# Products of a tile of ones on TensorE in the opening of a gated-attention and two-MLP kernel

## The reference, cut to what matters

```python
# attention, per batch (4) and head (8), 768 tokens, head size 48
for t in range(S):
    state = f[t][:, None] * state + outer(k[t], v[t])      # f = sigmoid(f_logit)
    y[t] = q[t] @ state
# first MLP on x (4, 768, 384): 384 -> 1536 -> 384, with a residual
xn = (x - mean) / sqrt(var + 1e-6) * g_ln
x = x + relu(xn @ w_ch1) @ w_ch2
# second MLP: 384 -> 1024 -> 384, with a gate from a convolution over 3 tokens
h = relu(x @ w_in)
out = (h * sigmoid(conv3(h, conv_w))) @ w_out
```

## Time and profile before

| | |
|---|---|
| median of 3 runs | 728.15 us (725.46 to 732.2) |
| the profiled execution | 729.54 us |
| its span, first to last instruction | 727.5 us |
| mean granted TensorE clock | 0.979 |
| TensorE busy in the span | 696.6 us (96%) |
| VectorE, ScalarE, GpSimd busy | 476.9, 311.6, 157.3 us |

### The profile page before, as it was taken

How to read it: one execution, slowest core, us unless ns; L and a number is a source line. 1 busy time by engine, 2 the same in 40 slices (tenths; PEclk the granted TensorE clock), 3 DMA queues, 4 the chain that set the end, 5 groups by cost and what they waited for, 6 DMA issues and landing times.

```text
span 727.5 us, 21762 instructions
## 1 busy us (share of the span) xinstructions
PE 696.6 (96%) x9616; PEld 651.1 (90%) x9616; DVE 476.9 (66%) x885; ACT 311.6 (43%) x604; POOL 157.3 (22%) x178
## 2 busy tenths in 40 slices
PE   4878899999999999999999999999999999999998
PEld 3556699999999999999999999999989999999997
DVE  2774886557765856765865863435387777777764
ACT  3262631341242251261151142224477676776764
POOL 4021503143333423423414414500000000000000
PEclk9769999999999999999999999999999999999999
DMA  8322520432152133332342112135010120220111
GB/s 330 128 99 97 180 90 3 186 121 100 59 196 108 59 128 116 120 121 90 106 170 88 57 57 88 57 103 179 33 38 31 45 75 1 75 75 1 37 39 38
DMA packets 23231, 67.71 MB, mean 93 GB/s; under 512 B 3809, under 2 KB 14817, under 8 KB 23137
## 3 DMA queue, kind: packets, MB, share of 16 engines
q1 hardware_dynamic: 23136, 66.32, 26.5%
HBM read 56.86 MB, written 9.45 MB: 91 GB/s over the span
## 4 chain that ended last, share of the span: by engine, by line
PE 90%; DVE 5%; issue 2%; DMA 2%; ACT 1%; SPq 0%; DVEq 0%; ACTq 0%
PE bank L1118 14%; PE bank L1120 13%; PE bank L1119 13%; PE bank L1313 9%; PE bank L1015 9%; PE bank L1315 9%; PE bank L1314 9%; PE bank L1037 4%; DMA F<-f 2%; PE bank L1089 2%; PE bank L1059 2%; PE bank L1031 1%; PE bank L951 1%; PE bank L1112 1%; PE bank L1100 1%
## 5 line engine op out<-in xcount | busy, mean ns | idle before, releaser
L705 ACT ACTIVATE HHI<-bank 128x384 fp32r<-128x384 f32 x96 | 47.2, 492 | 160.0 <-PE bank L1120 159.7
L1290 DVE SCALAR_TENSOR_TENSOR TB<-HB,CW,TB 128x440 f32<-128x440 f32 x112 | 75.8, 677 | 50.2 <-ACT TB L1253 48.2
L917 DVE SCALAR_TENSOR_TENSOR HLO<-bank,HHI 128x384 fp32r<-128x384 f32 x96 | 53.2, 554 | 83.7 <-ACT HHI L705 83.7
L1118 PE MATMUL bank<-HHI,W2H 128*128 128x384 f32 x288 | 100.6, 349 | 0.0
L1118 PE MATMUL bank<-XH,W1H 128*128 128x384 f32 x288 | 99.1, 344 | 0.0
L1120 PE MATMUL bank<-XH,W1L 128*128 128x384 f32 x288 | 96.5, 335 | 0.0
L1120 PE MATMUL bank<-HHI,W2L 128*128 128x384 f32 x288 | 96.5, 335 | 0.0
L1119 PE MATMUL bank<-XL,W1H 128*128 128x384 f32 x288 | 96.4, 335 | 0.0
L1119 PE MATMUL bank<-HLO,W2H 128*128 128x384 f32 x288 | 96.4, 335 | 0.0
L793 DVE TENSOR_TENSOR K<-K,TOT 128x768 f32<-128x768 f32 (+2 forms) x54 | 56.7, 1052 | 47.4 <-PE bank L1015 37.0
L1015 PEld LDWEIGHTS bank<-Q,K 48*64 48x64 f32 x3840 | 65.9, 144 | 22.0 <-issue 21.9
(11 more groups left out here) (127 smaller groups left out, 1373.5 us busy)
## 6 DMA issues: line engine op xcount, KB each, us to landing
NEAR<-near SPq DMA_DIRECT2D x21, 960.0 KB, 4.7
Q<-q SPq DMA_DIRECT2D x7, 768.0 KB, 4.3
K<-k SPq DMA_DIRECT2D x7, 768.0 KB, 4.9
F<-f SPq DMA_DIRECT2D x7, 768.0 KB, 6.1
V<-v SPq DMA_DIRECT2D x8, 576.0 KB, 6.9
x2d<-X SPq DMA_DIRECT2D x8, 576.0 KB, 4.4
XB<-x2d SPq DMA_DIRECT2D x6, 663.0 KB, 5.9
out<-OB SPq DMA_DIRECT2D x6, 660.0 KB, 4.4
```

The costliest lines, as they stand in the source:

```text
L705: nc.scalar.activation(HHI[:, g % RA], ub[g % 2][:, 0:T], ACT.Relu).then_inc(hh_ready, 1)
L917: nc.vector.scalar_tensor_tensor(out=HLO[:, g % RA], in0=ub[g % 2][:, 0:T], scalar=0.0, in1=HHI[:, g % RA].bitcast(F32), op0=ALU.max, op1= ...
L1118: mm(dst, ah, bh, start=start, stop=False, **kw)
L1290: nc.vector.scalar_tensor_tensor(out=TB[:, g % RB], in0=HB[:, g % RB, tap:tap + TB_], scalar=CW[:, g, tap:tap + 1], in1=TB[:, g % RB], op0 ...
```

## The change

`START` gets 36 `warm` steps, all of TensorE. Each consists of two products of 128x128 on 384 columns, but the first, in front of everything, of 20. Three steps stand behind each of `even0.a`, `even0.0` and `odd0.a`, two behind `odd0.0`, and two in front of each of the twelve `score` steps of unit 0 (`.a` and `.0`). All other steps keep their order. No wait is added but that of the first `warm` for `still_ready`. In all 90 products are added.

```diff
+        WARM_FIRST = 20
...
         START = placed("""
-            gates1.a gates1.0 even0.a whi0.0 diag0.0 even0.0 baseK0.a baseK0.0 baseQ0.a odd0.a baseQ0.0 pT0.a
-            odd0.0 whi1.0 pT0.0 self0.a wsub0.0 wlo0.0 wsub1.0 wlo1.0 score0.a wlo2.0 gates0.1 score0.0 pQ0.0
...
+            warm0.0 gates1.a gates1.0 even0.a warm1.0 warm2.0 warm3.0 whi0.0 diag0.0 even0.0 warm4.0 warm5.0
+            warm6.0 baseK0.a baseK0.0 baseQ0.a odd0.a warm7.0 warm8.0 warm9.0 baseQ0.0 pT0.a odd0.0 warm10.0
+            warm11.0 whi1.0 pT0.0 self0.a wsub0.0 wlo0.0 wsub1.0 wlo1.0 warm12.0 warm13.0 score0.a wlo2.0
+            gates0.1 warm14.0 warm15.0 score0.0 pQ0.0 wsub2.0 pQ0.a self0.0 pK1.a wsub3.0 gates1.1 warm16.0
+            warm17.0 score1.0 whi2.0 wsub4.0 warm18.0 warm19.0 score1.a whi3.0 pK1.0 warm20.0 warm21.0
+            score2.0 wlo3.0 copy3.0 pT1.a warm22.0 warm23.0 score2.a wsub5.0 whi4.0 warm24.0 warm25.0 score3.a
+            pT1.0 mask0.0 warm26.0 warm27.0 score3.0 mask0.a pQ1.0 pQ1.a baseK0.1 copy3.a near0.1 pK2.0 pT2.0
+            wlo4.0 mask1.0 pQ2.0 pK2.a pT2.a warm28.0 warm29.0 score4.0 mask1.a warm30.0 warm31.0 score4.a
+            pQ2.a pK3.0 pK3.a warm32.0 warm33.0 score5.0 mask2.a whi5.0 pT3.a pT3.0 warm34.0 warm35.0 score5.a
+            pQ3.a wsub6.0 ktr0.0 copy4.0 pQ3.0 wsub7.0 wlo5.0 mask2.0 pK4.a pK4.0 pT4.0 pT4.a pQ4.0 copy4.a
...
                 if i == 0:
                     pe.wait_ge(still_ready, 1)
-                for _ in range(2):
+                for _ in range(WARM_FIRST if i == 0 else 2):
                     mm(yb[:, 0:T], HLO[:, 0, 0:P], HLO[:, 0], start=True, stop=True)
```

More of the change, by code:

```diff
@@ L363, in phase_a @@
         START = placed("""
-            gates1.a gates1.0 even0.a whi0.0 diag0.0 even0.0 baseK0.a baseK0.0 baseQ0.a odd0.a baseQ0.0 pT0.a
-            odd0.0 whi1.0 pT0.0 self0.a wsub0.0 wlo0.0 wsub1.0 wlo1.0 score0.a wlo2.0 gates0.1 score0.0 pQ0.0
-            wsub2.0 pQ0.a self0.0 pK1.a wsub3.0 gates1.1 score1.0 whi2.0 wsub4.0 score1.a whi3.0 pK1.0
-            score2.0 wlo3.0 copy3.0 pT1.a score2.a wsub5.0 whi4.0 score3.a pT1.0 mask0.0 score3.0 mask0.a
-            pQ1.0 pQ1.a baseK0.1 copy3.a near0.1 pK2.0 pT2.0 wlo4.0 mask1.0 pQ2.0 pK2.a pT2.a score4.0 mask1.a
@@ L369, in phase_a @@
[L369 to L378, removed]
@@ L379, in phase_a @@
-            up2.0 pK5.1 up3.0 up4.0 neary1.1 baseK0.2 wlo13.0 ktr0.1 y0.1 pT5.1 xh1.0 gates1.2 copy3.1 pQ5.1
-            hlo0.0 baseQ0.2 kv0.1 pK6.1 xh2.0 pT6.1 pow0.1 hlo1.0 wlv9.0 hlo2.0 yend0.1 pQ6.1 sscale0.1
+            warm0.0 gates1.a gates1.0 even0.a warm1.0 warm2.0 warm3.0 whi0.0 diag0.0 even0.0 warm4.0 warm5.0
+            warm6.0 baseK0.a baseK0.0 baseQ0.a odd0.a warm7.0 warm8.0 warm9.0 baseQ0.0 pT0.a odd0.0 warm10.0
+            warm11.0 whi1.0 pT0.0 self0.a wsub0.0 wlo0.0 wsub1.0 wlo1.0 warm12.0 warm13.0 score0.a wlo2.0
@@ new lines, in phase_a @@
+            pQ2.a pK3.0 pK3.a warm32.0 warm33.0 score5.0 mask2.a whi5.0 pT3.a pT3.0 warm34.0 warm35.0 score5.a
+            pQ3.a wsub6.0 ktr0.0 copy4.0 pQ3.0 wsub7.0 wlo5.0 mask2.0 pK4.a pK4.0 pT4.0 pT4.a pQ4.0 copy4.a
+            wsub8.0 score0.1 baseQ0.1 y0.0 pK5.0 pQ4.a pT5.0 copy5.0 wlo6.0 kv0.0 pQ5.0 yend0.0 pK5.a wlo7.0
+            pT5.a pQ5.a pK6.0 ktok0.0 pK6.a pT6.0 pT6.a wlo8.0 neary0.1 copy5.a pQ6.a pQ6.0 wsub9.0 pT0.1
+            pQ0.1 nsum0.1 ktr1.0 wsub10.0 score1.1 pK1.1 wlo9.0 xadd0.0 ktok1.0 mask0.1 y1.0 pT1.1 kv1.0 pQ1.1
@@ new lines, in phase_a @@
+            yend1.0 wsub11.0 st0.0 xnt0.0 norm0.0 y2.0 wlo10.0 pow0.0 xadd1.0 pK2.1 sscale1.0 xn0.0 st1.0
+            mask1.1 pT2.1 sscale2.0 pQ2.1 xl0.0 gates0.2 yend2.0 xh0.0 score2.1 ktr2.0 whi6.0 wsub12.0 kv2.0
+            xadd2.0 wsub13.0 norm1.0 wsub14.0 xnt1.0 score3.1 wsub15.0 norm2.0 mask2.1 ktok2.0 xacc0.0 xnt2.0
+            pow1.0 xn1.0 pK3.1 st2.0 pT3.1 pQ3.1 pow2.0 near1.1 xacc1.0 xl1.0 xn2.0 score4.1 pK4.1 pT4.1
+            wlo11.0 up0.0 up1.0 pQ4.1 nsum1.1 xacc2.0 whi7.0 wlv8.0 score5.1 wlo12.0 azero0.2 whi8.0 xl2.0
@@ L381, in phase_a @@
+            down0.0 up2.0 pK5.1 up3.0 up4.0 neary1.1 baseK0.2 wlo13.0 ktr0.1 y0.1 pT5.1 xh1.0 gates1.2 copy3.1
+            pQ5.1 hlo0.0 baseQ0.2 kv0.1 pK6.1 xh2.0 pT6.1 pow0.1 hlo1.0 wlv9.0 hlo2.0 yend0.1 pQ6.1 sscale0.1
             wlo14.0 pT0.2 wlv10.0 hlo3.0 pQ0.2 down1.0 score0.2 wlo15.0 wlv11.0 down2.0 xadd0.1 whi9.0 st0.1
```

## The result

| | median | lowest to highest |
|---|---|---|
| changed kernel, 20 executions | 731.56 us | 729.16 to 736.18 |
| kernel before, 20 executions | 726.75 us | 724.16 to 732.20 |

The account below looks back on a forecast made before the run. TensorE, 90% of the chain, was taken to bound the kernel. Gains of 0.3, 2.5, 0.95 and 0.6 made 4.35 us, less 0.9 for holes, plus 0.5 at 57 us: 4.0 gained, median 724.1, range 718.5 to 735.5.

Parts of the forecast that it names:

- (c): From 25.8 to 38.65 us, TensorE alone: 12.85 us becomes 10.1, pairs 18 to 27 costing 3.4 of 6.1; gain 2.5.
- The 20 in front: Opening products, ending at 7.8 us under cover of the loads: cost nothing and raise the clock by 8 us.
- (a): From even0.0 at 10.68 us through odd0.0, which ends at 15.3 instead of 15.8: gain 0.3 us.
- (b): Up to 25.8 us, where VectorE sets the pace: pairs 10 to 17 are covered; without cover they would cost 2.7.
- The holes: Waits without a releaser in the short products, up to four of 0.45 us: 0 to 1.8 lost, 0.9 taken.
- the prediction's signs: List of what would show it right, among them fourth-level copies at 35.6 us and the dense part from about 82.7.
- (d): At score4.0: 1.97 us becomes 1.02, the pairs about it lying in waits for ScalarE and VectorE; gain 0.95.
- (f): Seventh weight split gains 1.1 us, but VectorE's Q for score0.1 is only 0.7 ahead: gain 0.6.
- (e): At score5: 48 short products fall by some 0.7 us and pair 34/35 costs 0.7: no gain.
- the low stretch at 57 us: Low clock from 57 to 60.2 us, no pair there: 0 to 1.6 us gained, 0.5 taken.
- The first: Rival: clock low for three tenths of (c) makes pairs lose; low at 10.68 us costs another 3.6; 738 us, chance 0.14.
- the ramp penalty: Low stretches across the opening, to 84.1 us: some 13 us by the rows, against 7.3 at most by the skill.

## Why the prediction was wrong

The place was right in the main: the end follows the start of the dense part (640.0 to 640.8 us long in the three profiles of this and of the kernel before, 639.9 to 643.4 in the experiments), and (c) got shorter. The sign was wrong. That the measured 731.56 lies between 718.5 and 735.5 is owed to the width of this range; the forecast within it was 724.1. Term by term:

**The 20 in front.** Costed at nothing; they end at 7.55, under the cover named, and the clock is high behind them, as forecast. Right by its mechanism. By themselves they bring no gain (1.0027).

**(a) and (b), gain 0.3 and nothing lost: a loss of 2.1 us at score1.0.** This is the first step that failed. Odd0.0 ends at 16.9 and not at 15.3. Six products take 1.31 us behind short ones and not 1.0, and the stream breaks for 0.69 us ahead of even0.0 and for 1.30 us inside odd0.0. Then the clock fell at 17, so that four products and a split run at half speed, and the chain stays on TensorE, holes included, until score0.0 ends at 24.4, where it had been VectorE's from 16 to 19.8: pairs 10 to 15, which (b) had covered, are on the path. The run without the token pairs starts score1.0 1.6 us earlier, but its time doesn't confirm the gain. With only score pairs, score1.0 starts at 26.5 instead of 26.1, so that (b) by itself was nearly right.

**The holes, 0 to 1.8 taken as 0.9.** Ahead of score0.1 the chain of the changed kernel has 3.2 us of them, against 0.9 in the earlier trace rows (0.48 and 0.45): 2.3 more, beyond the bound. I had them only in the score steps behind 28 us. The one in odd0.0 stands behind its 54th product in all four profiles with this order of instructions on 384 columns up to there (1.30, 0.76, 1.01 and 0.96 us: the changed kernel, and without 18 to 27, without 30 to 35, and without score pairs). The opening with 16 columns has the same order at the low clock and no hole there, and no other order or count has one in odd0.0. The falling of the clock at 17 is in two of these four.

**(c), gain 2.5: a gain of 1.6.** The mechanism and the sign are right, the size is off in two terms that partly cancel. The clock is worth 3.4 us there and not 6.1 (9.4 us with no product in it, VectorE being late next, by 0.76, 0.59 and 0.57 where I had 0.25). The pairs make (c) 1.8 us longer and not 3.4: the ten take 4.1 us of the chain, and VectorE's lateness hides the rest. That the net came within 1 us is luck. (By the sum 0.3 + 2.5 the copies would start at 35.9, not at the 35.6 of the prediction's signs.)

**(d) to (f), gain 1.55: a loss of 2.5.** The second step that failed, and the larger. The clock fell at 44.6, in a stretch of waits, and score4.0 has a hole of 1.22 us. The sum has a gap besides: (d) covers the pairs about score4 and (e) pays for 34 and 35, but 32 and 33, in front of score5.0, stand in no term, though TensorE waited only 0.41 us there. The four pairs stood between steps at 0.35 to 0.4 us a product. From the start of score4.a to the end of score5.a it is 5.5 us instead of 3.1. Taking out 30 to 35 takes away 2.5 to 2.8 of the 4.8 us, and 3.1 of the 4.0 at the seventh split. The clock was high from that split on and brought back 1.0 us, where (f) has 0.6.

**The base.** The profile I worked from is 2.6 us later at the dense part than the second one. From score0.1 on the difference lies in the low stretch at 57 us (some 1.5 by the chains) and in a longer hole ahead of it (2.32 against 1.15). I gave 0.5 for that stretch; the changed kernel has one of the same length, from 61.3 to 64.5, so nothing came of it. My median too, 728.15 of three executions, was 1.4 above that of twenty.

**The rivals.** The first (the clock does not hold, and the change is slower) had the sign, the price of a product and, for the token steps without the 20, the 3.6 us. Its point of decision, three tenths of (c) at the low clock, was not what decided: in the changed kernel's profile (c) was high throughout and the kernel slower all the same. In that profile the loss stands before and behind (c). The Trainium skill (TensorE: Matmul & The Clock Gate, What's actually happening) says that the ramp penalty is under 1% of a typical span and advises against fitting it; the rows made it 13 us, and I argued against the page. No run here takes the penalty away without putting products in its place, so none measures it. The products that held the clock at full from 20 to 51.5 us saved no time, and 3.4 us (0.5%) is the most that a stretch here showed, (c) in the run with pairs in front of waits.

What stays open: what makes the holes, and with it how much of the loss is theirs. Most come in streams of short products at the high clock, at an instruction that stays the same in kernels with the same steps ahead of it, and the opening with 16 columns, at the low clock, has none. That fits a fetch that can't keep up. But one of 0.70 us (only the 20, at 37.6) and the one of 2.51 (only 18 to 27) stand at the low clock, and with four products a step there is none up to 68 us, at the high clock; no run isolates the cause. The single steps don't add up either: the 20 alone +2.1, token pairs alone +4.6, score pairs alone +3.2, together +4.8, each within some 2 us; the clock's pattern is shared between them.

## What to carry to other kernels

Work that is there to hold the clock has a price on TensorE's path, and a yield which is bounded by what VectorE leaves of the stretch: work out the stretch at the high clock with the next engine's waits in it before counting the gain, and give every added product a term of the sum, also where it seems to be covered. Here one, two and four products a step cost 7.8, 4.7 and 7.9 us by the ratios: one product did not hold the clock, four held it and cost more than it gave. And take a second profile of the unchanged kernel first, since the clock's low stretches and the holes differ from execution to execution.

## What the runs showed of the hardware

- A product of 128x128 weights on 16 columns adds 0.23 us at the low clock and 0.14 at the high one, against 0.32 and 0.17 on 384. At the low clock six such products take 1.38 us and the loading of their weights 1.35: on so few columns the weights set the price.
- Products on 384 columns behind short ones with other shapes take more than 0.17 us: six 1.24 to 1.26 us on the chain, four 0.90 (0.70 behind a weight split, which has their shape), at the high clock.
- The granted clock column stood at 1.00 from the start although the clock was low: in the changed kernel the 20 take 0.31 us each under a column of 1.00.
- The unchanged kernel took 722.6 to 733.2 us over 94 executions. Of two with a profile, the slower by 3.4 us has a low stretch more behind 50 us and a longer hole ahead of it.
- A low stretch costs most where TensorE has no other engine to wait for: with only score pairs, 85 to 88 us at a clock of 0.50 lie in a dense part that takes 642.6 us instead of 640.0, with a hole of 0.81 in it.
